# Attention in groups of two tiles on one Trainium2 core: scores and V products alternate, two groups turn in one step, and four theta tiles run among the last groups

## What is computed

```python
# 1: attention with a window of 128 keys and 4 sinks (keys 0 to 3 are always seen)
scores = scale * q @ k.T                       # per head, 768 x 768
keep = is_sink | in_window                     # 0 <= row - column < 128
a = softmax(where(keep, scores, -1e9))
x = a @ v                                      # heads side by side: 768 x 512
# 2: a token mixer with turned phases
theta = x @ w_theta
y = w_tok_r @ (x * cos(theta)) + w_tok_i @ (x * sin(theta))
u = x + y
x2 = u + relu(u @ w_ch)
# 3: a gated MLP with a spatial product
h = relu(x2 @ w_in);  u, v = halves of h;  v = layernorm(v)
out = (u * (w_spatial @ v + b_spatial)) @ w_out
```

## Time and profile before

| | us |
|---|---|
| median of 3 runs | 460.03 (459.51 to 460.06) |
| the profiled execution, its own time | 460.16 |
| its span in the trace | 458.4 |
| PE busy | 433.2 (95%) |
| DVE busy | 226.4 (49%) |
| ACT busy | 168.9 (37%) |
| POOL busy | 189.4 (41%) |

### The profile page before, as it was taken

The page is one execution under the profiler, slowest core; times in us unless marked ns, Lnnn a source line. Parts: engine busy times, 40 slices in busy tenths (PEclk is TensorE's granted clock), DMA queues, the critical chain, the costliest instruction groups (busy, mean ns, idle before and its releaser), DMA issues.

```text
span 458.4 us, 7198 instructions
## 1 busy us (share of the span) xinstructions
PE 433.2 (95%) x2712; PEld 369.9 (81%) x2712; DVE 226.4 (49%) x468; ACT 168.9 (37%) x418; POOL 189.4 (41%) x130
## 2 busy tenths in 40 slices
PE   0899999999986999999999999999999999999997
PEld 0577777777665879999999997887887889999885
DVE  4548777777736798333223555616515403332222
ACT  2336566566523875333224104524223311111221
POOL 3499778883000018886674400000000164433442
PEclk9999999999997999999999999999999999999999
DMA  3744533431000002001200014000002000000222
GB/s 124 268 146 157 173 124 137 158 117 42 1 1 6 1 0 93 0 1 65 119 0 2 0 42 200 1 0 1 0 0 92 0 1 1 0 0 0 86 99 92
DMA packets 9444, 26.94 MB, mean 59 GB/s; under 512 B 1217, under 2 KB 2241, under 8 KB 9409
## 3 DMA queue, kind: packets, MB, share of 16 engines
q1 hardware_dynamic: 7776, 21.24, 13.1%
q0 software_dynamic: 1344, 5.24, 3.2%
q10 hardware_dynamic: 288, 0.00, 0.0%
HBM read 23.33 MB, written 3.15 MB: 58 GB/s over the span
## 4 chain that ended last, share of the span: by engine, by line
PE 92%; DVE 3%; ACT 2%; issue 1%; DMA 1%; POOL 0%; SPq 0%; ACTq 0%; DVEq 0%
PE ps L1075 23%; PE ps L1077 22%; PE ps L1076 22%; PE ps L1132 8%; PE ps L1093 8%; PE ps L1111 3%; PE ps L1139 2%; PE ps L1145 2%; DMA k_raw<-in_k_t 1%; PE ps L1113 1%; DVE x2l L996 0%; DVE x L993 0%; PE ps L1100 0%; ACT x2h L691 0%; POOL zl L468 0%
## 5 line engine op out<-in xcount | busy, mean ns | idle before, releaser
L1075 PE MATMUL ps<-tok_hi,zl 128*128 128x384 f32 x192 | 64.2, 335 | 0.2 <-POOL zl L468 0.2
L1077 PE MATMUL ps<-tok_hi,zh 128*128 128x384 f32 x192 | 64.1, 334 | 0.0
L1076 PE MATMUL ps<-tok_lo,zh 128*128 128x384 f32 x192 | 64.1, 334 | 0.0
L526 ACT ACTIVATE probs<-ps,neg_max 128x160 f32<-128x160 f32 (+1 forms) x96 | 37.3, 401 | 46.6 <-DVE neg_max L799 46.4
L468 POOL TENSOR_TENSOR zl<-cos_sb,zh 128x768 fp32r<-128x768 f32 x8 | 18.9, 2365 | 65.4 <-ACT zh L633 65.3
L970 DVE TENSOR_TENSOR x_t<-ps,x_t 128x768 f32<-128x768 f32 x16 | 15.3, 957 | 58.9 <-PE ps L1077 58.9
L1075 PEld LDWEIGHTS ps<-tok_hi,zl 128*128 128x128 f32 x192 | 36.0, 188 | 0.6 <-POOL zl L468 0.6
L500 POOL DMA_DIRECT2D wo_raw<-in_moe_w_out x1 | 0.8, 785 | 86.1 <-PE ps L1077 86.1
L1076 PEld LDWEIGHTS ps<-tok_lo,zh 128*128 128x128 f32 x192 | 36.0, 188 | 0.0
L1077 PEld LDWEIGHTS ps<-tok_hi,zh 128*128 128x128 f32 x192 | 36.0, 188 | 0.0
L495 POOL TENSOR_TENSOR vl<-vn_sb,vh 128x768 fp32r<-128x768 f32 x8 | 19.6, 2446 | 37.2 <-ACT vh L683 37.2
(11 more groups left out here) (150 smaller groups left out, 1140.4 us busy)
## 6 DMA issues: line engine op xcount, KB each, us to landing
tok_raw<-in_w_tok SPq DMA_DIRECT2D x6, 768.0 KB, 7.5
k_raw<-in_k_t SPq DMA_DIRECT2D x8, 464.0 KB, 5.7
q_raw<-in_q_t SPq DMA_DIRECT2D x8, 384.0 KB, 4.2
v_raw<-in_v_p SPq DMA_DIRECT2D x8, 384.0 KB, 2.9
out<-o_sb SPq DMA_DIRECT2D x12, 256.0 KB, 2.0
sp_raw<-in_w_sp SPq DMA_DIRECT2D x3, 768.0 KB, 5.9
in_raw<-in_moe_w_in POOLq DMA_DIRECT2D x1, 2048.0 KB, 8.5
th_raw<-in_moe_w_theta POOLq DMA_DIRECT2D x1, 1024.0 KB, 5.7
```

The lines of the kernel that those rows point to most:

```text
L526: act.activation(probs[i % 2][:, cols, h], s_ps[i % 2][:, h, cols], ACT.Exp, bias=neg_max[:, i % 2, h:h + 1], accum_out=sums[:, i, h:h + 1 ...
L1075: pe.matmul(dst, w_lo, m_hi, start=first, stop=False)
L1076: pe.matmul(dst, w_hi, m_lo, start=False, stop=False)
L1077: return pe.matmul(dst, w_hi, m_hi, start=False, stop=last)
```

## The change

- Work goes in 24 groups of two tiles. In step s PE does `scores(2s)`, `times_v` of group s-2 (both tiles), `scores(2s+1)`, `turn_probs` of group s-1 (both tiles) and `turns(s-2)`. ACT and DVE get matching orders, written out in full instead of in a loop on ACT.
- `turn_probs` of a group makes four transposes and one for the sinks of both tiles (full width). For that `probs` becomes one tensor in which the four columns (two tiles by two heads) alternate element by element, and `v_sink` gets one set of rows for each tile of a group; it is twice as large in the transfer.
- Results are turned in twos: `turns(g)` transposes the two output tiles of group g and the two normalised tiles of group g-1 in one go, with one semaphore.
- DVE takes both maxima of a tile in one instruction, and adds the epsilon from a constant tensor.
- Four theta tiles instead of two are made among the last groups, ahead of the branch; tiles 2 and 3 have slots of their own for `xth` and `xtl`.
- The theta results go to PSUM banks in another order, POOL splits a piece of the token weights ahead of making `v_d`, and the clearing of a PSUM bank at the start is replaced by one of two columns of `probs`.

PE in the middle of the attention, before: one tile and the turn behind it. `p_t` and `p_d` are the turned probabilities and their masked copy.

The diff, cut to its core:

```diff
-        probs = [at(f"probs{b}", o + 6144 + 8 * FOLD * b, [P, FOLD, 2], F32) for b in range(2)]
+        probs = at("probs", o + 8192, [P, 2, FOLD, 4], F32)
...
-            return banks[(0, 2, 3, 1, 2, 3)[t // 2]][:, t % 2, :]
+            return banks[(0, 1, 2, 3, 1, 2)[t // 2]][:, t % 2, :]
...
 # ACT
+            for step in range(GROUPS):
+                exps(2 * step)
+                if step >= 2:
+                    copy_o(step - 2)
+                if step >= 1:
+                    copy_pt(2 * step - 2)
+                exps(2 * step + 1)
+                if step >= 1:
+                    copy_pt(2 * step - 1)
...
 # DVE
+                dve.tensor_reduce(neg_max[:, i % 2, :], s_ps[i % 2][:, :, cols], AX.X, ALU.max, negate=True).then_inc(s_max, 1)
...
+            for step in range(GROUPS + 2):
+                if step >= 3:
+                    normalise(step - 3)
+                if step >= 4:
+                    copy_x(step - 4)
+                if step < GROUPS:
+                    maxima(2 * step)
+                if 2 <= step:
+                    diagonal(2 * step - 3)
+                if step < GROUPS:
+                    maxima(2 * step + 1)
+                if step >= GROUPS:
+                    for t in range(2 * (step - GROUPS), 2 * (step - GROUPS) + 2):
+                        x_low(t)
+                if step >= 2:
+                    weights(step - 2)
+                if 1 <= step <= GROUPS and step % HALVES != 1:
+                    diagonal(2 * step - 2)
+            normalise(GROUPS - 1)
+            copy_x(GROUPS - 2)
+            copy_x(GROUPS - 1)
...
 # PE
+            def turn_probs(g):
...
+                for j in range(2):
+                    pe.wait_ge(s_exp, 4 * g + 2 * j + 2)
+                    for h in range(2):
+                        pe.transpose(pt_ps[:, j, h * P:(h + 1) * P], probs[:, g % 2, 0:P, 2 * j + h], ident[:, :])
+                pe.transpose(pt_ps[:, 0, WIN:WIN + P], probs[:, g % 2, P:FOLD, :].rearrange("p s j -> p (s j)"),
+                             ident[:, :]).then_inc(s_pt, 1)
...
+            for step in range(GROUPS):
+                scores(2 * step)
+                if step >= 2:
+                    times_v(step - 2)
+                scores(2 * step + 1)
+                if step >= 1:
+                    turn_probs(step - 1)
+                if step >= 2:
+                    turns(step - 2)
+            times_v(GROUPS - 2)
+            turn_probs(GROUPS - 1)
+            turns(GROUPS - 2)
             pe.wait_ge(s_th_w, 2)
-            pe.wait_ge(s_exp, 2 * (2 * PAIRS * TILES - 1))
             theta(0)
-            times_v(2 * PAIRS * TILES - 1, TILES - 1, 2 * PAIRS - 1, PAIRS - 1, 1)
+            times_v(GROUPS - 1)
             theta(1)
-            turn_o(2 * PAIRS - 1, 1)
-            turn_x(2 * PAIRS - 1, PAIRS - 1, 1, 1)
+            turns(GROUPS - 1)
+            pe.wait_ge(s_exp, 2 * ALL_TILES)
+            theta(2)
+            turns(GROUPS)
+            theta(3)
```

More of the change, by code:

```diff
@@ L36 @@
 FOLD = P + SINKS
+THETA_EARLY = 4
 SCALE = 1.0 / math.sqrt(HD)
@@ L208, in attn_moe_gmlp @@
         s_ps = banks[0:2]
-        pt_ps = [banks[2][:, b, :] for b in range(2)]
+        pt_ps = banks[2]
         o_ps = banks[3][:, 0, :]
@@ L602, in _ @@
                 act.wait_ge(s_g_free, GT * PAIRS + 1)
[L604 to L605 removed]
+                for j in range(THETA_EARLY):
+                    act.activation(xth[xt_slot(j)][:, :, :], x_t[:, :, j * P:(j + 1) * P], ACT.Copy).then_inc(s_g_xth, 1)
                 act.wait_ge(s_g_theta, 1)
@@ L1130, in times_v @@
+            def times_v(g):
+                no, n, b, i = place(2 * g)
+                pe.wait_ge(s_v[b], 32 * (n + 1))
+                if g:
+                    pe.wait_ge(s_oc, g)
+                pe.wait_ge(s_vd, no + 1)
+                for j in range(2):
+                    t = i + j
+                    cols = slice(j * P, (j + 1) * P)
+                    pe.wait_ge(s_ptc, 2 * g + j + 1)
                     for h in range(2):
                         rows = slice(h * HD, (h + 1) * HD)
-                        mm = pe.matmul(o_ps[rows, cols], values[:, rows], turned[h], start=(j == 0), stop=(j == len(parts) - 1))
@@ new lines, in times_v @@
+                    if t:
+                        for h in range(2):
+                            rows = slice(h * HD, (h + 1) * HD)
+                            pe.matmul(o_ps[rows, cols], v_sink[b][:, j, rows], p_t[:, 0, WIN:WIN + P], start=False, stop=False)
+                        pe.wait_ge(s_ptd, diagonals(no, t))
+                        for h in range(2):
+                            rows = slice(h * HD, (h + 1) * HD)
+                            mm = pe.matmul(o_ps[rows, cols], v_d[b][:, t - 1, rows], p_d[:, j, h, :], start=False, stop=True)
@@ new lines, in times_v, with turns @@
+                mm.then_inc(s_pv, 1)
+            def turns(g):
+                if g >= 1:
+                    pe.wait_ge(s_norm, g)
+                if g >= 2:
+                    pe.wait_ge(s_xt, g - 1)
+                if g < GROUPS:
+                    pe.wait_ge(s_oc, g + 1)
+                    for j in range(2):
+                        mm = pe.transpose(tr_ps[:, j * P:(j + 1) * P], x_raw[g % 2][:, j, :], ident[:, :])
+                if g >= 1:
+                    _, n, b, i = place(2 * (g - 1))
+                    for j in range(2):
+                        mm = pe.transpose(tr_ps[:, (2 + j) * P:(3 + j) * P], x_sb[:, b * TILES + i + j, n * P:(n + 1) * P],
+                                          ident[:, :])
+                mm.then_inc(s_turn, 1)
@@ L1251, in token_block @@
                     pe.wait_ge(s_u, turn - 1)
+                if turn == 1:
+                    for half in range(2):
+                        pe.wait_ge(s_theta_used[half], 5)
                 pe.wait_ge(s_zl, turn + 1)
```

328 lines of the change are left out of this document (115 added, 213 removed).

## The result

The changed kernel is slower: 467.3 us (median of 4 runs, 465.56 to 469.11) against 459.77 (4 runs), a ratio of 1.0196, 95% interval 1.015 to 1.0243. 455.3 was predicted, with a range of 448 to 463.5. The profiled execution was the slowest of the four, 469.11 us, with a span of 466.9. Medians in this document are over all executions of a kernel, and ratios over those within 1.5% of its fastest, which leaves out one of eight in run 8 and five of twelve in run 12.

The account below looks back on a forecast made before the run. PE, busy 95% of the span, was taken as the bound, with DVE's chain binding mid attention after the change. Gains of 1.2 + 0.1 + 0.3 + 0 + 3.2 = 4.8 us gave a 455.3 us median, range 448 to 463.5.

Parts of the forecast that it names:

- `weights` two short ones, 0.36: In DVE's chain for a group in mid attention: two short `weights` instructions, priced at 0.36 us together.
- The chain that the prediction had itself named as the binding one: Mid attention: DVE's chain to `p_d`, 4.34 us, which PE waits for; 4.75 us per group.
- Pairs 0 and 1: Early attention at the lower clock, PE the bound: 1.2 us gained, bounds 0.5 lost to 3.6 gained.
- Five pairs: Mid attention: 13.45 us per pair against 13.47, 0.1 us gained; bounds 7.4 gained, 3 lost.
- The mechanism, PE behind the second group of `p_d`: Mid attention: PE waits for DVE's masked copy of the odd tile, idling about 0.7 us a group.
- Pair 7 to the end of theta tile 1: End of attention, 24.0 us before: 0.3 us gained, bounds 1.5 either way.
- To DVE's first theta work: From the end of theta tile 1, 7.4 us before and 7.4 after: nothing gained.
- From there to the token block: From DVE's first theta work to the first token block: 25.4 us against 28.66, 3.2 gained.
- The sum: Whole kernel: 4.8 us gained, 455.4 us profiled and 455.3 as a median.
- R1: Rival: strided `probs` weight loads slow `turn_probs` by 0.4 us each, 6.9 us in all, 462.3 us; chance 0.25.
- R2: Rival: PE's clock falls or rises late, 458 to 463 us, chance 0.15; an early rise gives 453.
- R3: Rival: DVE's chain doesn't bind in mid attention, PE's 4.0 us per group holds, 447.9 us; chance 0.10.

Follow-up runs that it names:

- run 8: Run 2 with the old `probs` layout: element step of 8 bytes, sink columns turned tile by tile, sink products over 64 rows; 463.34 us, ratio 1.010.
- run 12: The kernel before, with POOL's split of the theta weights moved behind its last V step; 460.60 us, ratio 0.999.
- Run 1: The changed kernel with DVE's addition of 1e-9 (`den`) left out, the reciprocal reading the sums; 455.63 us, ratio 0.993.
- run 2: The changed kernel with the addition `den` done by ACT, behind the group's exponentials; 455.23 us, ratio 0.993.
- run 11: Run 5 with ACT's copy of V's output ahead of the exponentials and POOL's theta weight split behind its last V step; 443.83 us, ratio 0.971.
- Run 6: Run 2 with theta tiles 2 and 3 put back behind the branch on PE; 459.23 us, ratio 1.002.
- run 9: Run 5 with `probs` at an element step of 8 bytes, PE's work unchanged, the output's sink weights wrong; 450.74 us, ratio 0.986.
- run 5: Run 2 with `p_d` of the second tile moved ahead of the maxima in DVE's order; 450.94 us, ratio 0.984.
- run 7: The changed kernel with DVE's addition and reciprocal moved behind the second `p_d`; 470.18 us, ratio 1.023.

## Why the prediction was wrong

*The step that failed* is "`weights` two short ones, 0.36", inside DVE's chain. It was priced at the length that these instructions have when POOL rests. The 23 records of `den` until 142 us take 15.5 us; at 0.15 each they would take 3.5. Run 1, without them and without the three falls of the clock, takes 11.7 us less than the changed kernel (455.63), which is 0.3 from the forecast. Stalls and falls don't simply add up, since they would be 17: of the stalls, 8.1 us show as waits of PE.

The chain that the prediction had itself named as the binding one is what made the stall matter: whatever stands in it must be priced with what else runs. The trace of before had the number, 161/504/1549 ns, and the prediction has no term for it.

*Pairs 0 and 1*, 1.2 gained: in run 1 pair 2 starts at 43.65 against 44.83, 1.2 gained; in run 2 at 41.56, 3.3 gained, with a clock that rose 10 us sooner. So the agreement in run 1 is luck. With `den` 2.3 were lost.

*Five pairs*, 13.45 each: 13.66 without `den`, 15.6 with it. The mechanism, PE behind the second group of `p_d`, was right (5.3 us in 14 waits in runs 1 and 2); the size was 0.2 a pair short. It came close by two errors that partly cancel: PE waits 0.5 us in two groups of three and not 0.7 in each, and its own work is more than 4.0, since run 11, with almost no waits left, still takes 12.43 a pair, 4.14 a group.

*Pair 7 to the end of theta tile 1*, 23.7 from its first scores: 149.05 less 124.76, 24.3. *To DVE's first theta work*, 7.4: 6.9. *From there to the token block*, 25.4: 24.6. Run 6 gives 3.0 for the early tiles, a fall of the clock among them, where 3.2 stood.

*The sum* of 455.3 is what the kernel takes once `den` is out of DVE's way: 455.63 and 455.23. Part of that is luck: in run 1 the five pairs lose 1.0 us where 0.1 gained stood, the first stretch of the end 0.3 where 0.3 gained stood, and the rest of the end gives 1.4 more than forecast.

*R1* fell on PE: a load of 212 against 200 ns is hidden, and only 3 of the 12 ns go with the step (209 in run 9). Its cost came out on ACT instead and was worth 0.1 us a pair in run 9.
The Trainium skill (SBUF — State Buffer, Specifications (TRN2)) wants two hits to each line of 16 bytes. For TensorE's load the trace shows almost nothing of it, for ScalarE's write 547 against 400 ns.

*R2* happened in part: the clock rose sooner (32.1 against 34.8 us, which says little, see run 12) and fell three times. Those falls go with the stalls: run 1, without them, has none. A fall was put at 2.6 us; these cost 1.7 each. *R3* did not: DVE's chain binds, and run 5 is what it takes to loosen it.

The forecast named its own failure rightly: pairs outside 12.8 to 14. It had no rival for a stall on DVE.

## What to carry to other kernels

Before work is moved into a chain that binds, look up the longest record of each of its instructions in the old trace, not the shortest: a maximum ten times the minimum on four or six elements meant here that it waited for another engine, and slack had been paying for it. On DVE, keep short instructions with two SBUF operands, and scalar forms on SBUF, out of such a chain while POOL is busy; ACT did the same addition in 0.22 us. Then order the chain's engine by who waits: one swap on DVE gave 0.8 us a pair and one on ACT 0.4.

## What the hardware showed that was not expected

- An addition on 4 or 6 elements a partition took 0.15 to 4.12 us: beside a running POOL instruction it ended when that one did, whether it was a subtraction or a CAST. A reciprocal of one SBUF operand (165 to 173 ns in run 1) and products with one operand in PSUM didn't wait.
- ACT's exponential over 160 columns takes 400 ns with an element step of 8 bytes and 547 with 16; PE's weight load takes 200 to 209 and 212.
- A 64-row product between 128-row products costs PE about 0.15 us at each change, an estimate from 2.06 against 1.46 us with four changes a group.
- In 12 of the 15 profiles here the clock fell to 1.2 GHz inside the work, mostly for 3.4 or 6.8 us, in or behind a wait of PE of 0.98 to 4.1 us. The length of the wait doesn't tell: 2.23 us in run 7, 2.19 in run 2 and 1.73 in run 1 kept 2.4 GHz, while in the changed kernel falls came behind waits of 0.98. In run 12 it fell for 13.7 us behind a wait of 1.88. Why once for 3.4 us and once for 13.7 is open.
- When the clock first rises differs by more than 10 us between profiles of kernels with the same early work (22.9 us in run 2, 33.1 in run 1), and with it the start of pair 2 by 2 us.
